# Two doubling levels in one pass of 96 columns: four of five level passes of a linear-attention kernel become two

## The reference

```
for t in range(S):                                   # linear attention with a decay per channel
    y[t]  = r[t] @ (state + u * outer(k[t], v[t]))
    state = w[t][:, None] * state + outer(k[t], v[t])
h = x @ w_in;  x = (max(h, 0) ** 2) @ w_out          # 384 -> 2048 -> 384
e = argmax(x @ w_gate);  p = softmax(...)[e]         # 8 experts, at most 384 tokens for each
y = p * (max(x @ w1[e], 0) @ w2[e])                  # 384 -> 1024 -> 384, rows of one expert together
```

## Time and profile before

| | us |
|---|---|
| median of 3 runs | 451.7 (450.69 to 452.8) |
| the profiled execution | 451.77 |
| its span, first to last instruction | 450.0 |
| outside of the span | 1.77 |
| PE busy | 428.6 (95%) |
| PEld busy | 406.7 (90%) |
| DVE busy | 303.2 (67%) |
| ACT busy | 257.7 (57%) |
| POOL busy | 63.4 (14%) |

### The profile page before, as it was taken

One profiled execution on the slowest core, in us unless ns is written; L12 is line 12 of the kernel. 1 busy time (PEld: TensorE's weight loads), 2 busy tenths in 40 slices (PEclk: granted clock), 3 DMA queues, 4 the chain that ended last, 5 costly groups with the idle time before them and its releaser, 6 DMA issues.

```text
span 450.0 us, 14551 instructions
## 1 busy us (share of the span) xinstructions
PE 428.6 (95%) x5882; PEld 406.7 (90%) x5882; DVE 303.2 (67%) x763; ACT 257.7 (57%) x527; POOL 63.4 (14%) x88
## 2 busy tenths in 40 slices
PE   3799999999999999999999999999999899999994
PEld 3678999999999999999999999989998789999994
DVE  6797866766777767777778638568548867687510
ACT  3366766546654664466446665573638766686421
POOL 8700000000000100010001000301031323421201
PEclk9999999999999999999999999999999989999999
DMA  7837886850400131010001093613785989520001
GB/s 240 300 102 244 309 296 243 308 225 3 167 31 1 39 133 65 3 37 2 4 1 39 2 358 136 204 60 94 284 297 165 353 280 300 172 62 2 30 2 45
DMA packets 35643, 63.40 MB, mean 141 GB/s; under 512 B 3980, under 2 KB 21950, under 8 KB 35568
## 3 DMA queue, kind: packets, MB, share of 16 engines
q1 hardware_dynamic: 33120, 57.87, 37.9%
q0 software_dynamic: 2304, 4.47, 2.7%
q10 hardware_dynamic: 144, 0.00, 0.0%
HBM read 50.77 MB, written 14.19 MB: 144 GB/s over the span
## 4 chain that ended last, share of the span: by engine, by line
PE 86%; POOL 3%; issue 3%; ACT 2%; DVE 2%; DMA 1%; POOLq 0%; SPq 0%; DVEq 0%; ACTq 0%
PE bank L767 22%; PE bank L753 22%; PE bank L980 6%; PE bank L933 5%; PE pair L672 5%; PE pair L634 4%; PE pair L948 3%; PE bank L948 3%; PE pair L933 3%; PE bank L987 3%; PE pair L693 2%; PE pair L728 1%; DMA stage<-in_moe_w_in 1%; PE pair L705 1%; PE pair L980 1%
## 5 line engine op out<-in xcount | busy, mean ns | idle before, releaser
L753 PE MATMUL bank<-XH,W 128*128 128x256 f32 x576 | 118.7, 284 | 0.1
L767 PE MATMUL bank<-W,GH 128*128 128x384 f32 x372 | 98.3, 345 | 0.2 <-issue 0.2
L753 PEld LDWEIGHTS bank<-XH,W 128*128 128x128 f32 x576 | 94.9, 189 | 1.1 <-issue 0.4
L753 PE MATMUL bank<-XL,W 128*128 128x256 f32 x288 | 80.6, 280 | 0.0
L1321 DVE TENSOR_TENSOR GL<-GG,GH 128x256 fp32r<-128x256 f32 x96 | 40.4, 421 | 35.1 <-ACT GH L1019 34.8
L1123 ACT ACTIVATE RB<-bank 128x256 f32<-128x256 f32 x96 | 36.6, 381 | 47.6 <-PE bank L753 47.1
L767 PEld LDWEIGHTS bank<-W,GH 128*128 128x128 f32 x372 | 61.7, 188 | 1.6 <-issue 0.4
L767 PE MATMUL bank<-W,GL 128*128 128x384 f32 x186 | 62.6, 336 | 0.0
L1019 ACT ACTIVATE GH<-GG 128x256 fp32r<-128x256 f32 x96 | 40.2, 418 | 34.1 <-PE bank L767 32.3
L753 PEld LDWEIGHTS bank<-XL,W 128*128 128x128 f32 x288 | 54.3, 189 | 0.0
L1256 DVE TENSOR_TENSOR KS<-KS 128x512 f32<-128x512 f32 (+1 forms) x72 | 48.9, 680 | 7.4 <-PE pair L672 7.2
(11 more groups left out here) (165 smaller groups left out, 733.6 us busy)
## 6 DMA issues: line engine op xcount, KB each, us to landing
raw<-in_moe_w SPq DMA_DIRECT2D x23, 768.0 KB, 7.1
stage<-in_moe_w SPq DMA_DIRECT2D x9, 768.0 KB, 8.0
KS<-in_krw SPq DMA_DIRECT2D x12, 512.0 KB, 5.2
slots<-X SPq DMA_DIRECT2D x8, 579.0 KB, 7.8
VV<-in_v SPq DMA_DIRECT2D x12, 288.0 KB, 5.5
KS<-in_krw SPq DMA_DIRECT2D x12, 256.0 KB, 5.3
stage<-in_moe_w_in SPq DMA_DIRECT2D x4, 768.0 KB, 5.9
stage<-in_moe_w_out SPq DMA_DIRECT2D x4, 768.0 KB, 5.6
```

What stands on the lines that cost most here:

```text
L753: last = nc.tensor.matmul(bank[4 + f % 2][:, 0:2 * P], win[wa][:, c, f * P:(f + 1) * P], xa[:, c, :], start=n == 0, stop=n == 3 * KM - 1)
L767: last = nc.tensor.matmul(bank[6 + m][:, 0:DM], ga[(NF * g + f) % G3][:, cols], wout[wa][:, f, :], start=f == 0 and n == 0, stop=f == NF - ...
```

## The change

Groups 1 to 5 do levels 1+2 in one pass and levels 3+4 in one pass (`PAIRS`; where levels are counted from one these are 2+3 and 4+5). The pass of a pair has the keys of its lower level as weights (62 or 56 columns, and 64 for the first one of group 1), and 96 moving columns: for each four runs of L, runs 1, 2, 3 as they are, and runs 2, 3, 3 out of `MIX` with decays that VectorE has multiplied on ahead of the pass (`reads_ahead`, two TENSOR_TENSOR per tile, of 256 and 128 elements). Of the 96 scores VectorE takes three parts under a new mask `mask4` (`select_pair`: 384, 256 and 128 elements, each waiting for the one before), where it took 256 and 256. `update` and `next_totals` stay for every level. GpSimd builds `mask4` behind its first work.

The table of slots, the slots of five weight splits, and the gate's slots of groups 0 to 2 are new. The first pair stands in slot 2, the second in slot 6; slots 1, 3, 5 and 7 hold no pass. Group 3 keeps the gate slots 7 to 9, group 4 keeps 11 to 13. PE no longer waits for `sel` ahead of `ranks`, and level 0 of tile 0 waits for `rank_used`.

```diff
-    PAGE_PAD = 160
+    PAGE_PAD = 176
-    LATER = (-1, 1, 3, 5, 7, 9, 10, 11, 12, 13)
+    LATER = (-1, 2, 3, 6, 7, 9, 10, 11, 12, 13)
+    PAIRS = (1, 3)
-    LOW_SLOT = (5, 6, 7, 18, 20, 22, 26, 29)
+    LOW_SLOT = (5, 6, 7, 17, 21, 24, 26, 29)
-    GATE_SLOT = (None, None, 23, 24, 25)
+    GATE_SLOT = (None, None, 28, 29, 30)
+    THIRD_LAST = (None, None, 23, 24, 25)
...
+            step(nc.gpsimd.memset(wide4[:, :, :], 1.0))
...
+            nc.gpsimd.tensor_tensor(mask4[:, :, :], wide4[:, :, 0:3 * C // 4], wide4[:, :, 3 * C // 4:3 * C // 2],
+                                    ALU.add).then_inc(masked, 1)
...
+                if t == 0:
+                    need(pe, rank_used, i - 3)
...
+            def two_levels(i, t, l):
+                L = 1 << l
+                pe.wait_ge(ahead[t], 4 * (i - 1) + 2 * PAIRS.index(l) + 2)
+                pe.wait_ge(sel[t], NMASK * i + l)
...
+                n = C if (i, l) == (1, PAIRS[0]) else C - L
...
+                            reads = bass.AP(first.tensor, first.offset,
+                                            [first.ap[0], [apart, 2], [4 * L, C // (4 * L)], [1, 3 * L]])
+                            last = nc.tensor.matmul(pair[t][to:to + n, a, q * P:q * P + 3 * C // 2],
+                                                    x[rows, XW + c:XW + c + n], reads, start=q == 0, stop=q == HP - 1)
+                last.then_inc(att[t], 2)
...
-                    elif k < NL:
+                    elif k < NL and (n == 0 or k == NL - 1):
                         level(n, t, k)
+                    elif k in PAIRS:
+                        two_levels(n, t, k)
...
-                        if attn:
-                            pe.wait_ge(sel[0], NMASK * (i + 1))
                         ranks(g)
...
+            def select_pair(i, t, l):
...
+                take(1, 4, 0, 0).then_inc(part_sel[t], 1)
+                dve.wait_ge(part_sel[t], done + 1)
+                take(2, 4, 1, 0).then_inc(part_sel[t], 1)
+                dve.wait_ge(part_sel[t], done + 2)
+                take(3, 4, 1, 2).then_inc(sel[t], 2)
+
+            def reads_ahead(i, t, l):
...
+                tt(got[:, :, 1:3, :], x[:, :, 2:4, :], td[:, :, 1:3, :].to_broadcast([P, XW // (4 * L), 2, L]),
+                   ALU.mult).then_inc(ahead[t], 1)
+                dve.wait_ge(ahead[t], done + 1)
+                tt(got[:, :, 3, :], got[:, :, 2, :], td[:, :, 1, :].to_broadcast([P, XW // (4 * L), L]),
+                   ALU.mult).then_inc(ahead[t], 1)
...
                 next_totals(n, t, k)
+                if n > 0 and k + 1 in PAIRS:
+                    reads_ahead(n, t, k + 1)
```

More of the change, by code:

```diff
@@ L116, in rwkv_moe_kernel @@
         mask2 = IN[0][0][:, :, :].rearrange("p h n -> p (h n)")[:, 0:NMASK * C].rearrange("p (l n) -> p l n", l=NMASK)
-        mask = sb("mask", [P, NMASK, C // 2], on=p1)
+        mask = sb("mask", [P, NMASK - 1, C // 2], on=p1)
+        mask4 = sb("mask4", [P, 2, 3 * C // 4], on=p1)
         eye = sb("eye", [P, C], on=p1)
-        U = sb("U", [P, HP], on=p1)
         empty = X2[:, 0, :]
         X2B = sb("X2B", [P, 2, ROW], on=p1)
+        wide4 = X2B[:, 0, 0:3 * C].rearrange("p (l n) -> p l n", l=2)
+        low = X2B[:, 1, 0:C // 2]
         p1.close()
@@ L224, in rwkv_moe_kernel @@
         tot = [sem(f"tot{n}") for n in range(2)]
+        ahead = [sem(f"ahead{n}") for n in range(2)]
+        part_sel = [sem(f"part_sel{n}") for n in range(2)]
         sel = [sem(f"sel{n}") for n in range(2)]
@@ L527, in to_row, with folded @@
                                                pattern=[[2 * L, C // L], [0, L]], channel_multiplier=-1)
[L529 to L531 removed]
+            def folded(to, lo, hi):
+                return nc.gpsimd.tensor_tensor(to, mask2[:, lo:hi, 0:C // 2], mask2[:, lo:hi, C // 2:C], ALU.add)
             step(from_row(0))
@@ L536, in _ @@
             pool.wait_ge(cst, n_cst[0])
-            step(folded(0, 1))
+            step(folded(low.rearrange("p (l n) -> p l n", l=1), 0, 1))
             pool.wait_ge(cst, n_cst[0])
             odd = right_half(eye[:, :], 0)[:, :, 0]
-            nc.gpsimd.tensor_tensor(odd, odd, mask[:, 0, :], ALU.add).then_inc(made, 1)
+            nc.gpsimd.tensor_tensor(odd, odd, low, ALU.add).then_inc(made, 1)
             for l in range(1, NMASK):
@@ L546, in _ @@
             pool.wait_ge(cst, n_cst[0])
-            folded(1, NMASK).then_inc(masked, 1)
+            folded(mask[:, :, :], 1, NMASK).then_inc(masked, 1)
             def first_totals(t, l):
@@ L675, in level @@
                 last.then_inc(att[t], 1)
+            def two_levels(i, t, l):
+                L = 1 << l
+                pe.wait_ge(ahead[t], 4 * (i - 1) + 2 * PAIRS.index(l) + 2)
+                pe.wait_ge(sel[t], NMASK * i + l)
+                x = KRW[t][i % 2]
+                apart = (2 - i % 2) * WIDTH - XW
+                n = C if (i, l) == (1, PAIRS[0]) else C - L
+                for q in range(HP):
+                    for h in range(2):
+                        for a in range(2):
+                            rows, c = slice(DP * a, DP * a + D), q * P + h * C
+                            to = half(h, a).start
+                            first = x[rows, c + L:c + L + 1]
+                            reads = bass.AP(first.tensor, first.offset,
[3 more added lines that the diff above has]
+                last.then_inc(att[t], 2)
             def kk_rows(i, t):
@@ L1451, in step @@
                 else:
-                    if k < NMASK:
+                    if n > 0 and k in PAIRS:
+                        select_pair(n, t, k)
+                    elif n == 0 and k < NMASK:
                         select(n, t, k)
```

43 lines of the change are left out of this document (38 added, 5 removed).

## The result

The changed kernel takes 455.53 us (median of 4 runs, 455.28 to 455.71), the kernel before 451.61 beside it: a ratio of 1.0085, 95% interval 1.0061 to 1.0109. It is slower by 3.9 us, or 0.85%, and the interval leaves out 1. The forecast was 445.2, the range 442.0 to 450.0, and slower had 0.07.

The account below looks back on a forecast made before the run. PE's queue was taken to bound the kernel, busy for 184.00 of 184.00 us in groups 2 to 5. Sum: 451.8 - 8.3 (passes) + 0.9 (group 1) + 0.8 (gate) = 445.2 us, range 442.0 to 450.0.

Parts of the forecast that it names:

- The scatter's buffer: Gate's new place: the buffer is wanted again four slots on; cost 0, or 0.4 a time if ACT waits.
- VectorE's copies at 461.2: Rival: score copies take 2.3 us a triple at both pairs, making the kernel slower, 461.2 us; chance 0.05.
- the two row halves at 461.1: Rival: weight loads overlap only across two row halves, so a 96-column pass takes 2.88 us, 461.1 in all; chance 0.02.
- Passes: Groups 1 to 5: two 96-column passes at 1.3 us replace four, saving 1.65 us a group, 8.3 in all.
- the upper bound: 96-column pass: if each quarter loads and streams in turn, 1.48 us a pass, saving 6.5 us in all.
- The low bound: 96-column pass keeps the old pace, 1.04 us, bound by loads; as a rival 442.6 us, chance 0.10.
- Place (a): PE's `project` of slot 5 needs VectorE's GL of slot 3; GL was to come some 0.4 us early, costing nothing.
- The second rival: VectorE eats more: group 1 gains nothing, 0.6 us lost at either near place in groups 2 to 5; 448.4, chance 0.17.
- (b): Level 5's pass needs tile 1's update of level 4 from VectorE; it was to come 0.4 us early, costing nothing.
- Group 1: Weight splits stand between the passes there, so only some 0.8 of the 1.65 us is left: 0.9 lost.
- Gate's place: Gate work in slot 14 delays XL for level 0's pass: 0.4 us in iterations 3 and 4, 0.8 lost; ends 0 and 2.4.
- Code placement: Rival: expert stage has one more 1.61 us wait, 448.4 us, chance 0.05; or loses the present one, 442.0, chance 0.03.

Follow-up runs that it names:

- after_again: The changed kernel, unaltered, measured again beside the kernel before on one chip: 456.24 us, ratio 1.0080 to the kernel before.
- held_again: The changed kernel with the first two scatters held until level 0's pass of the next group is over, measured again: 450.33 us, ratio 0.9947 to the kernel before.
- scatter_held: The changed kernel with GpSimd's scatters of groups 0 and 1 held until level 0's pass of the next group has ended: 449.86 us, ratio 0.9938.
- moved_held: The kernel before with the gate in slots 12 to 14 and the scatter held, without pairs or new split slots: 454.03 us, ratio 1.0042.
- plain_dma: The changed kernel with the scatter held, plus two plain DMAs of the same rows by SyncE beside level 0's pass: 450.22 us beside 451.73.

## Why the prediction was wrong

The step that failed is "The scatter's buffer is wanted again four slots on; cost 0, and 0.4 a time if ACT has to wait." It priced the scatter by its buffer alone, and didn't ask what it would run beside. The gate is one chain, and its end, GpSimd's scatter, moved five slots with it, onto level 0's pass of groups 4 and 5. That costs 5.9 us in the comparison. In the first profile it is 2.0 + 1.9 us of stall and 1.6 of low clock; in the second profile of the same kernel it is 2.0 + 1.8, and the clock stayed at 1.00 behind it. The rest of the 5.9 fits the clock of the other executions: the median of their mean granted clocks is 0.990 for after_again and 0.9965 for held_again, and 0.0065 of 450 us is 2.9 us, an estimate of what that can cost at most. None of the rivals had the scatter: the two that ended on the slower side, VectorE's copies at 461.2 and the two row halves at 461.1, are both refuted by the triples of 1.55 and 1.35 us and the passes of 1.48.

With the scatter held the kernel takes 450.33 beside 453.04: 2.7 faster, where 6.5 were forecast (451.7 to 445.2). The rest, step by step:

- **Passes.** 1.3 was taken, 1.48 measured, the upper bound (each quarter loads and streams in turn): 2 x 0.18 a group, 1.8 in five groups. 1.19 by streaming alone was nearly right for the slope (13.3 ns a column of a pass, 12.4 taken). What was missing is a fixed 0.2 us. The saving per group is 4.61 - 2 x 1.66 = 1.3, as the bound said. The low bound fell: from 64 columns on every column costs. By the rule of the Trainium skill ("TensorE: Matmul & The Clock Gate", The mechanism), that weight loads go beside a running matmul only in another row group, a pass would have taken 2.88, the prediction's estimate; the measured 1.48 does not agree with it.
- **Place (a).** 0.4 early was forecast, 0.24 late (group 5: 0.48) measured, 1.2 us in four groups. The second rival put 0.6 a group there or at (b). At (b) nothing waits. The copies are the reason: 1.55 instead of 1.3 in the first pair, two tiles, 0.5 of the 0.65 by which it misses.
- **Group 1.** 0.8 of gain was left; measured is none: its stretch lasted 44.50 before, and 44.55 (scatter_held), 45.13 (the first profile after) and 45.94 us (held_again) with the pairs. The first wait is one that the prediction hadn't in its list: PE, with less work in slots 1 to 4, comes ahead of weights that still arrive by DMA, and ScalarE splits them first (1.44, 2.08 and 1.55 in these three). It isn't the pairs' alone: moved_held, without them, waits 1.00 at the same place, the kernel before not at all. Then 1.0 for GL behind the first pair's copies, which the prediction had named as a sign. The spread has two sources: in the first profile after, the granted clock was 0.50 from 45.00 to 47.00, behind the wait of 2.08, and GL then held nobody up; held_again has the stop of 1.05 at 64.99.
- **Gate's place.** 0.8 was forecast, 1.0 measured by medians (453.04 to 454.03) and 1.9 by the ratio (0.5 to 3.4). Ahead of level 0 only half of that stands, 1.37 us instead of 1.15 from the start of the last `project` rows in `scatter_held`, two times; where the rest is stays open. The VectorE order came out as described:

```profile
163.92 0.17 DVE L1476 TENSOR_REDUCE small<-ex 128x2 f32<-128x16 f32 x1 [0.86 <-ACT ex L1146]
...
165.01 0.43 DVE L1403 TENSOR_TENSOR GL<-GG,GH 128x256 fp32r<-128x256 f32 x1
...
166.09 1.02 DVE L1398 TENSOR_TENSOR XL<-pair,XH 128x384 fp32r<-128x384 f32 x2
```

- **Third scatter.** "0.4 a time if ACT has to wait" had been counted as 0: it waits in iteration 6, 0.41 us for PE in the profile after and 0.82 in held_again.
- **Code placement.** The one wait of 1.61 stayed in kind: 2.29 for VectorE's weight split at 362.67, without the slow matmuls behind it: there the granted clock is 1.00, in the profile before it was 0.50 from 359.09 to 362.50.

The pairs' own balance by these terms: 8.3, less 1.8 for the passes, less group 1's 1.3 that never came, less 1.2 at (a): 4.0. Measured: 3.7, with the new split slots in it; with the splits in their old slots only 1.9 are left (454.03 - 452.17). That the forecast of 0.8 for the gate came near its 1.0 is partly luck, since half of it isn't where the prediction put it.

## What to carry to other kernels

When a chain is moved, follow it to its last instruction and look at what each engine does at that time in the new place; an asynchronous transfer at the end has a neighbour too, not only a buffer. A wait that holds such a transfer back by 2 us can be worth more than the passes saved: here 5.9 us against 3.7. And where one engine bounds the kernel, taking work from it brings it ahead of its suppliers in the stretch where they are late anyway (group 1), so price that stretch at zero gain.

## What the runs showed of the hardware

- Two indirect scatters of 128 rows, issued in a row by GpSimd, stop PE in a dense pass of quarter-array matmuls in fp32 (15 to 17 ns a record): three gaps and 1.8 to 2.0 us for level 0's pass of 1.09, two gaps and 1.1 to 1.7 us for the outputs' pass of 0.97, with the first gap always behind 39 to 45 records. Eight MEMSETs on GpSimd or 288 GB/s of plain DMA do nothing; one scatter does 0 to 0.2 us; a pass of 23 ns a record isn't touched; nor are `hidden` and `project` beside the scatters of the kernel before. Which resource is shared isn't shown. That PE's instructions arrive too slowly would fit with the pace and with the nearly constant number of records ahead of the first gap, but no run measures it.
- A dense pass can also stop without a scatter: three profiles (held_again, after_again, plain_dma) have one gap of 1.05 to 1.09 us in group 1's state outputs, with no instruction on GpSimd, and others have none. Its cause is open.
- The granted clock fell to 0.54 for 3.5 us behind one such stall (PE busy for 1.97 of 3.10 us), and stayed at 1.00 behind the stall of group 5 in the same profile and behind both stalls in another profile of the same kernel.
- Quarter-array passes have a floor of 1.05 us for 64 records up to 64 columns, and cost 13.3 ns a column above (1.90 us at 128).
- COPY_PREDICATED in three parts of 384, 256 and 128 elements takes 1.55 us with a base run of two elements and 1.35 with one of eight.
